# Attention, MoE, MoE: token rows scattered to one region per expert in place of a computed permutation

## The chip, the cores and the metric

The kernel is one program on one core of a Trainium2 chip. Its time is the time of one execution on the device, in microseconds (us). The engines are TensorE (PE; its weight loads are listed apart as PEld), VectorE (DVE), ScalarE (ACT), GpSimd (POOL) and SyncE (SP). They run their own instruction streams and meet at semaphores only. DMAs are issued from the streams of SP, ACT and POOL.

## The reference

All data are float32. N = 4 x 768 = 3072 tokens, DM = 8 heads x 64 = 512, E = 8 experts, F = 1024.

```python
x = attention(q, k, v)              # 4 batches, 8 heads; local window of 96, 8 global keys, a bias by distance
# first MoE
logits = x @ w_gate;  e = argmax(logits)
gate = softmax(logits)[e];  eom = sigmoid(x @ w_output_gate)[e]
x2 = gate * eom * (relu(x @ w1[e]) @ w2[e])
# second MoE
logits = normalise(x2) @ normalise(expert_emb).T / tau;  e = argmax(logits)
out = softmax(logits)[e] * (relu(x2 @ w1[e]) @ w2[e])
```

Each token goes to one expert, so the work of a layer is that of all token tiles (128 rows each), with every expert's count rounded up to whole tiles: 29 tiles in the first MoE and 28 in the second, for these inputs.

## The kernel before

**Attention.** The tokens are 24 tiles of 128 rows, six to a batch. `attention_steps` calls `step(b, u)` on PE, DVE and ACT, software-pipelined: 12 values of `u` for a batch, two for a tile (`j = u // 2`). The first batch's steps and the last ones are written out, batches 1 to 3 are a loop. In a step PE makes scores, transposes the probabilities, and multiplies them by V; DVE adds the bias (`nbias`) and takes the minimum; ACT takes the exponentials and copies transposed tiles. At the end of a tile PE transposes the sums (`x_transposes`) and multiplies by both gates (`gate_logits`), DVE normalises into `x_tok` (two buffers) and adds up the 16 logits of each token into `logits`, and ACT issues the store of the tile's rows to `x_rows` in DRAM (L727).

**Route.** After the last tile, `route` on DVE works on all tiles at once: the argmax as a one-hot array, counts, the gate weight of each token, each token's rank within its expert (PE, L1217 to L1221, with the triangular matrix `before` and with `ones`), and each token's place in the order by experts. That permutation is then inverted: 24 (second layer: 32) pairs of one-hot tiles go through PE (L1228), and what comes out is, for each slot, the token that it holds (`gather_i`), its scale (`scale_c`) and in the second layer the row that it is written to (`scatter_i`). `tab` holds the tile at which each expert ends.

**Experts.** The tiles then run expert by expert. For tile i: POOL gathers 128 rows by index into `x_g` (L632); PE transposes them (`x_tr`, L1126), DVE copies them to `x_gt` (L1064); `first_product` is 64 matmuls (L1246) into four banks, which ACT clears with ReLU into `h_t` (L777); `second_product` is 16 matmuls (L1256) into bank 4, which DVE scales into `y_sb` (L1075). The order on PE is

```python
first_product(i)       # waits for x_gt of tile i
x_tr(i + 1)
second_product(i)      # waits for h_t, and for y_sb of tile i - 1
```

so the transposition and the copy of the next tile lie under the second product. In the first layer ACT stores `y_sb` to `y_rows` and takes the squares for the norm, and DVE takes eight dot products with the expert embeddings (L1083, `next_logits`), from which `route` starts again. In the second layer POOL scatters `y_sb` to the output (L651). SP loads the weights: two experts are held at a time, and expert e + 2's first matrix is fetched as soon as expert e's last first product is done, its second one after the last second product.

Where a branch's condition fails (other sizes of the window), a general path with loops of its own is taken; it does not run here.

## Time and profile before

| | |
|---|---|
| median of 3 runs | 1151.79 us (1151.33 to 1152.15) |
| the profiled execution's own time | 1149.39 us |
| its span, first to last instruction | 1147.0 us |
| PE busy | 1061.3 us (93%) |
| DVE, ACT, POOL busy | 446.4, 262.9, 158.6 us |
| mean granted TensorE clock | 0.962 of full speed |

The profile is of one execution. The span is some 2 us shorter than the time that the device reports for it. A busy PE means that matmuls were in flight. Lines such as L1246 are lines of the kernel before.

### The profile page before, as it was taken

To read this page: it belongs to the slowest core of one execution; us is meant where nothing else is said; L and a number is where in the kernel's file an instruction comes from. 1 tells how busy PE (TensorE), PEld (TensorE's weight loads), DVE (VectorE), ACT (ScalarE), POOL (GpSimd) and SP (SyncE) were. 2 spreads that over 40 slices of the span, in tenths; PEclk is the share of its full clock that TensorE was granted. 3 is DMA by queue.
4 is the path that set the end of the run, shared out by engine and by line. 5 is a ranking of instruction groups with operands and counts; after the bars stand their busy time and mean duration, and the time that the engine had idled before them with its cause. 6 is when DMAs were issued, how large, how long until landed. Compare 5 with 4: busy or idle time off the path is not lost.

```text
span 1147.0 us, 20797 instructions
## 1 busy us (share of the span) xinstructions
PE 1061.3 (93%) x6936; PEld 806.0 (70%) x6936; DVE 446.4 (39%) x1541; ACT 262.9 (23%) x792; POOL 158.6 (14%) x437
## 2 busy tenths in 40 slices
PE   5999999848999999999999983799999999999995
PEld 4878888646777777777777763577777777777773
DVE  6777777662444444444444449100001111111110
ACT  4677677421111111111111110011111111111110
POOL 2010001001111111111111100122222222222221
PEclk9999999958999999999999995899999999999998
DMA  9865569211151542325151532015523235230110
GB/s 180 183 159 145 132 160 322 99 58 37 37 183 37 183 135 85 131 89 183 37 183 37 183 106 95 28 37 179 181 107 112 98 116 180 90 122 31 37 37 12
DMA packets 119861, 130.30 MB, mean 114 GB/s; under 512 B 80079, under 2 KB 80079, under 8 KB 119696
## 3 DMA queue, kind: packets, MB, share of 16 engines
q1 hardware_dynamic: 103456, 91.24, 26.8%
q0 software_dynamic: 6960, 21.77, 5.8%
q10 hardware_dynamic: 9408, 16.81, 4.0%
q8 instruction: 22, 0.36, 0.1%
q14 instruction: 15, 0.12, 0.0%
HBM read 103.58 MB, written 22.02 MB: 110 GB/s over the span
## 4 chain that ended last, share of the span: by engine, by line
PE 83%; issue 5%; DVE 5%; ACT 4%; DMA 1%; ACTq 1%; POOL 0%; POOLq 0%; DVEq 0%; SPq 0%
PE bank L1246 35%; PE bank L1256 34%; PE bank L1126 6%; PE bank L1199 2%; PE bank L1166 2%; PE bank L1228 2%; PE bank L1141 2%; ACT probs L709 2%; ACT q_t L687 1%; ACT y_two L721 1%; ACTq L727 1%; DVE neg_s L904 0%; DVE nbias L840 0%; DMA n_words<-in_n_local_dram 0%; DMA x_g<-x_rows,gidx 0%
## 5 line engine op out<-in xcount | busy, mean ns | idle before, releaser
L1246 PEld LDWEIGHTS bank<-x_gt,w_sb 128*128 128x128 f32 x3648 | 419.1, 193 | 28.7 <-issue 26.3
L1246 PE MATMUL bank<-x_gt,w_sb 128*128 128x128 f32 x3648 | 419.7, 276 | 1.6 <-DVE x_gt L1064 1.6
L1256 PE MATMUL bank<-w_sb,h_t 128*128 128x512 f32 x912 | 400.8, 592 | 0.0
L1256 PEld LDWEIGHTS bank<-w_sb,h_t 128*128 128x128 f32 x912 | 168.8, 190 | 190.8 <-issue 190.8
L777 ACT ACTIVATE h_t<-bank 128x256 f32<-128x256 f32 x228 | 86.8, 381 | 524.4 <-PE bank L1246 524.4
L1075 DVE TENSOR_SCALAR y_two<-bank,scale_c 128x512 f32<-128x512 f32 x57 | 42.8, 751 | 359.5 <-PE bank L1256 359.5
L586 POOL TENSOR_TENSOR pad_p<-zeros 128x1 f32<-128x1 f32 x196 | 36.9, 188 | 824.8 <-PE bank L1126 470.9
L1064 DVE COPY x_gt<-bank 128x512 f32<-128x512 f32 x59 | 40.8, 691 | 247.2 <-PE bank L1126 247.2
L1083 DVE CUSTOM_DVE_ANT_0 v_win<-y_two,nbias 128x512 f32<-128x512 f32 x174 | 108.8, 687 | 1.2
L785 ACT ACTIVATE y_two<-y_two 128x512 f32<-128x512 f32 x29 | 18.3, 631 | 246.4 <-DVE y_two L1075 246.4
L904 DVE CUSTOM_DVE_ANT_0 neg_s<-bank,nbias 128x256 f32<-128x256 f32 x192 | 70.3, 421 | 7.8 <-issue 6.0
L709 ACT ACTIVATE probs<-neg_s,neg_m 128x256 f32<-128x256 f32 x96 | 47.6, 497 | 51.1 <-DVE neg_m L904 51.1
L1166 PE MATMUL bank<-k_t,q_t 64*128 64x256 f32 x384 | 56.5, 414 | 2.7 <-DVE neg_m L904 1.5
L709 ACT ACTIVATE h_t<-neg_s,neg_m 128x256 f32<-128x256 f32 x96 | 47.7, 498 | 11.4 <-DVE neg_m L904 11.4
L1126 PE MATMUL bank<-ident,x_g 128*128 128x128 f32 x236 | 36.4, 278 | 14.9 <-DMA x_g<-y_rows,gidx 7.5
L1166 PEld LDWEIGHTS bank<-k_t,q_t 64*128 64x128 f32 x384 | 34.3, 192 | 13.7 <-issue 9.9
L1126 PEld LDWEIGHTS bank<-ident,x_g 128*128 128x128 f32 x236 | 28.2, 144 | 15.2 <-issue 15.2
L1083 DVE CUSTOM_DVE_ANT_0 q_in<-y_two,nbias 128x512 f32<-128x512 f32 x58 | 37.7, 687 | 0.0
L632 POOL DMA_INDIRECT x_g<-x_rows,gidx x30 | 31.4, 1045 | 16.0 <-issue 16.0
L632 POOL DMA_INDIRECT x_g<-y_rows,gidx x29 | 30.6, 1055 | 15.7 <-issue 15.7
L1126 PE MATMUL bank<-ident,probs 128*128 128x128 f32 x192 | 27.0, 285 | 5.9 <-ACT y_two L721 5.5
L1126 PEld LDWEIGHTS bank<-ident,probs 128*128 128x128 f32 x192 | 21.3, 144 | 15.6 <-ACT y_two L721 11.7
(176 smaller groups left out, 717.0 us busy)
## 6 DMA issues: line engine op xcount, KB each, us to landing
w_sb<-in_moe_w_dram SPq DMA_DIRECT2D x32, 2048.0 KB, 9.3
y_rows<-y_two ACTq DMA_DIRECT2D x29, 256.0 KB, 2.0
q_in<-in_q_dram SPq DMA_DIRECT2D x24, 256.0 KB, 3.8
k_in<-in_k_dram SPq DMA_DIRECT2D x24, 256.0 KB, 5.0
v_own<-in_v_dram SPq DMA_DIRECT2D x24, 256.0 KB, 3.4
x_rows<-x_tok ACTq DMA_DIRECT2D x24, 256.0 KB, 3.8
v_win<-v_own SPq DMA_DIRECT2D x20, 192.0 KB, 3.4
nbias<-in_moe_expert_emb_dram ACTq DMA_DIRECT2D x1, 2048.0 KB, 7.4
```

Of the source, the lines that this page charges most:

```text
L586: nc.gpsimd.tensor_tensor(pad_p[:, at:at + 1], zeros[:, 0:1], zeros[:, 0:1], ALU.add)
L632: nc.gpsimd.indirect_dma_start(out=x_g[:, :], out_offset=None, in_=src[:, :], in_offset=bass.IndirectOffsetOnAxis(ap=gidx[:, 0:1], axis=0) ...
L709: e_ = nc.scalar.activation(probs_of[u % 2][:, 2 * k + i, :], neg_s[:, k, i, :], ACT.Exp, bias=neg_m[:, i, s % STEPS:s % STEPS + 1], scale ...
L777: nc.scalar.activation(h_t[:, k * FPP:(k + 1) * FPP, :].rearrange("p c t -> p (c t)"), banks[k][:, 0:FPP * P], ACT.Relu).then_inc(L.h, 1)
L904: V.tensor_tensor_reduce(neg_s[:, k, i, :], score_banks[i][:, k * WIN:(k + 1) * WIN], nbias[:, c, 2 * (2 * half + k) + i, :], 1.0, 3e38, A ...
L1064: V.tensor_copy(x_gt[:, :, :].rearrange("p c t -> p (c t)"), banks[5][:, :]).then_inc(L.xt, 1)
L1075: V.tensor_scalar(y_sb, banks[4][:, :], scale_c[:, n, bass.ds(i, 1)], None, ALU.mult).then_inc(L.y, 1)
L1083: t_ = V.tensor_tensor_reduce(dot_out[e], y_sb, emb[:, e * DM:(e + 1) * DM], 1.0, 0.0, ALU.mult, ALU.add, dot[:, e:e + 1])
L1126: t_ = T.transpose(bank[:, c * P:(c + 1) * P], src[:, c * P:(c + 1) * P], ident[:, :])
L1166: m_ = T.matmul(score_banks[i][:, k * WIN:(k + 1) * WIN], q_t[rows, j % 2, 2 * half + k, :], k_t[rows, j % 2, 2 * half + k, :], start=True ...
L1246: m_ = T.matmul(banks[k][:, f * P:(f + 1) * P], w1_sb[:, w1 + c * FF + at:w1 + c * FF + at + P], x_gt[:, c, :], start=(c == 0), stop=(c == ...
L1256: m_ = T.matmul(banks[4][:, :], h_t[:, c, :], w2_sb[:, w2 + c * DM:w2 + (c + 1) * DM], start=(c == 0), stop=(c == FC - 1))
```

## The change

The rows of x are no longer stored in token order and gathered. DRAM has two arrays `bins` of one region (`CAP` rows) for each expert, and a row is 532 numbers: the 512 of x, then the token's scores and its number. While attention runs, DVE takes the argmax of three tiles at a time (`group_hot`), PE ranks their tokens (`group_ranks`), counting on from the groups before, and the rank plus the start of the expert's region is the row to which POOL scatters each token (`scatter_group`). The counts at the end give the tables (`tables`). Every region is filled up with zero rows behind its last token (`fill_bin`), and SP reads contiguous rows, in two DMAs of 64 rows for a tile. The scale of a tile's tokens is worked out when the tile is there, from the scores that came with its rows, on ACT (`gate_exps`) and DVE (`gate_weights`). In the first layer the same is done tile by tile for the next one: the scores are taken from the dot products (`next_scores`), PE ranks one tile (`rank_rows`), DVE makes the row numbers (`y_rows`) and POOL scatters (`bin_row`). The copy to `x_gt` moves from DVE to ACT, the loads of the weights from SP to ACT, and the expert loops of DVE and ACT are written out eight times, once for each expert. `route`, the permutation and the stores to `x_rows` and `y_rows` are gone.

The core of the diff (the general path, names and constants are left out):

```diff
+        def group_hot(dve, q, g, tile0):
...
+            link(V.tensor_scalar(own[:, :, ID_COL], ident_id[:, bass.ds(tile0, GROUP)], 0.0, None, ALU.add))
+            link(V.tensor_copy(g_pre[:, 0, :], g_pre[:, GROUP, :]))
+            link(V.tensor_reduce(g_min[:, :], neg, AX.X, ALU.min))
+            link(V.tensor_tensor(g_cmp[:, :, :], neg, wide(g_min[:, :]), ALU.is_equal))
+            link(V.tensor_tensor(g_cmp[:, :, :], g_cmp[:, :, :],
+                                 desc.unsqueeze(1).to_broadcast([P, GROUP, E]), ALU.mult))
+            link(V.tensor_reduce(g_min[:, :], g_cmp[:, :, :], AX.X, ALU.max))
+            link(V.tensor_tensor(g_hot[:, :, :], g_cmp[:, :, :], wide(g_min[:, :]), ALU.is_equal))
+            for m in range(GROUP):
+                ins = V.tensor_tensor(g_pre[:, m + 1, :], g_pre[:, m, :], g_hot[:, m, :], ALU.add)
...
+        def scatter_group(pool, hold_pool, q, g):
+            pool.wait_ge(s_pos, q + (1 + FIRST))
...
+            for m in range(GROUP):
+                nc.gpsimd.indirect_dma_start(
+                    out=bins[0][:, :], out_offset=bass.IndirectOffsetOnAxis(ap=sc_i[:, j:j + 1], axis=0),
+                    in_=x_tok[:, j, :], in_offset=None,
...
 # SP
+                for e in range(0, E, 2):
+                    fill_bin(sp, n, e)
+                def load_x(at, low, high):
+                    sp.wait_ge(L.xt, at + FIRST)
+                    sp.dma_start(x_g[0:UNIT, :], low).then_inc(L.x_ld, 16)
+                    sp.dma_start(x_g[UNIT:P, :], high).then_inc(L.x_ld, 16)
...
 # POOL, first layer
+                def bin_row(i):
+                    pool.wait_ge(L.y, i + (1 + FIRST))
+                    nc.gpsimd.tensor_copy(y_row[:, 0:DM], y_sb).then_inc(L.yc, 1)
+                    pool.wait_ge(L.yc, i + (1 + FIRST))
+                    pool.wait_ge(L.pos, i + (2 + FIRST))
...
 # ACT
-                t = j - 3
-                if half == 0 and exists(b, t, TPB):
-                    act.wait_ge(x_done, since(TPB * b + t + 1))
-                    act.dma_start(x_rows[bass.ds(b * S + t * P, P), :], x_tok[:, t % 2, :])\
-                        .then_inc(x_st[t % 2], 16)
...
+                def x_copy(i):
+                    act.wait_ge(L.x_ld, 32 * i + 32)
+                    act.wait_ge(L.t1, i + 1)
+                    act.wait_ge(L.mm1, MARKS * i + FIRST)
+                    act.wait_ge(L.sc, i + FIRST)
+                    nc.scalar.activation(pay[:, bass.ds(i + 1, 1), :].rearrange("p o c -> p (o c)"), x_g[:, DM:], ACT.Copy)
+                    nc.scalar.activation(x_gt[:, :, :].rearrange("p c t -> p (c t)"), banks[5][:, :],
+                                         ACT.Copy).then_inc(L.xt, 1)
...
+                for e, start, end in expert_spans(act, n):
+                    with act.Fori(start, end) as i:
+                        relu_full(i)
+                        gate_exps(i, e)
+                        x_copy(i + 1)
+                        if n == 0:
+                            squares(i)
+                    at = n * E + e + 2
+                    if at < 2 * E:
+                        act.wait_ge(L.mm1, MARKS * end + FIRST)
+                        load_w(act, at // E, at % E)
+                        act.wait_ge(L.mm2, end + FIRST)
+                        load_w2(act, at // E, at % E)
 # DVE (gate_weights, first layer)
+                        dve.wait_ge(L.ex, i + (1 + FIRST))
+                        chain(V.tensor_scalar(g_tmp4[:, 1:2], e_sum[:, :], 1e-9, None, ALU.add))
+                        chain(V.scalar_tensor_tensor(out=g_tmp4[:, 2:3], in0=e_sig[:, :], scalar=1.0,
+                                                     in1=g_tmp4[:, 1:2], op0=ALU.add, op1=ALU.mult))
+                    V.reciprocal(scale[:, :], g_tmp4[:, 2:3]).then_inc(L.sc, 1)
...
+                def y_rows(i):
+                    dve.wait_ge(L.rank, i + 1)
+                    ids = pay[:, bass.ds(i, 1), 2 * E:2 * E + 1].rearrange("p o c -> p (o c)")
+                    chain(V.tensor_tensor(cmp1[:, :], banks[6][:, 0:E], hot1[:, :], ALU.mult))
+                    chain(V.tensor_reduce(r1[:, 0:1], cmp1[:, :], AX.X, ALU.add))
+                    chain(V.tensor_scalar(r1[:, 1:2], ids, 0.0, OFF, ALU.is_equal, ALU.mult))
+                    V.tensor_tensor(sidx[:, :], r1[:, 0:1], r1[:, 1:2], ALU.add).then_inc(L.pos, 1)
...
+                for e, start, end in expert_spans(dve, n):
+                    with dve.Fori(start, end) as i:
+                        here(i)
+                        if n == 0:
+                            y_rows(i)
+                        gate_weights(i, e)
+                        y_full(i)
+                        if n == 0:
+                            next_scores(i)
...
 # PE
+                def rank_rows(i):
+                    pe.wait_ge(L.hot, i + FIRST)
+                    pe.wait_ge(L.pos, i + FIRST)
+                    T.matmul(banks[6][:, 0:E], before[:, :], hot1[:, :], start=True, stop=False)
+                    T.matmul(banks[6][:, 0:E], ones[:, :], pre1[:, :], start=False, stop=True).then_inc(L.rank, 1)
...
                     with pe.Fori(start, end) as i:
+                        first_full(i, w1)
                         x_tr(i + 1)
+                        second_full(i, w2)
+                        if n == 0:
+                            rank_rows(i)
```

`first_full` and `second_full` are the two products as they were. `L.sc` starts at `FIRST` (1) and rises by one for each tile's `gate_weights`; `L.rank` starts at 0. `chain` and `link` make DVE wait for its own instruction before the next one; in `chain` the value waited for is worked out from the loop's register.

## Rows read from the trace of the kernel before

**Rows 1.** The page: chain that ended last, shares by engine and line.

```profile
PE 83%; issue 5%; DVE 5%; ACT 4%; DMA 1%; ACTq 1%; POOL 0%; POOLq 0%; DVEq 0%; SPq 0%
```

**Rows 2.** Stretches: length, busy PE, PEld, DVE, ACT, POOL, clock, DMA share, GB/s.

```profile
150.00:180.00 30.00, 29.28 (x297) 24.40 (x292) 22.43 (x99) 20.30 (x69) 2.60 (x9) 1.00 0.63 151
...
226.00:244.00 18.00, 1.87 (x6) 1.78 (x6) 11.53 (x47) 7.86 (x20) 0.00 (x0) 0.51 0.33 133
...
280.00:685.00 405.00, 404.82 (x2353) 297.28 (x2351) 188.27 (x588) 59.99 (x168) 41.60 (x108) 1.00 0.33 114
```

**Rows 3.** Chain that ended last, whole kernel: start us, length us, what.

```profile
263.97 8.95 PE bank L1246 x64
...
540.32 7.14 PE bank L1246 x64
547.90 6.87 PE bank L1256 x16
...
677.95 6.88 PE bank L1256 x16
...
728.36 8.86 PE bank L1246 x64
```

**Rows 4.** The same chain, in the two gaps between the stages.

```profile
226.07 2.85 issue
...
231.72 2.47 issue
...
256.60 0.30 POOLq L625
...
258.38 3.62 DMA x_g<-x_rows,gidx
...
687.23 0.61 DVE v_win L1083
```

**Rows 5.** Timeline: small instructions and hand-overs, in and beside the gaps.

```profile
234.40 0.22 ACT L759 ACTIVATE r_rows<-r_rows 128x24 f32<-128x24 f32 x1 [4.11 <-DVE r_rows L965]
...
263.22 0.69 DVE L1064 COPY x_gt<-bank 128x512 f32<-128x512 f32 x1 [5.90 <-PE bank L1126]
...
701.38 0.43 PE L1221 MATMUL bank<-r_cum,ones 128*128 128x8 f32 x2
701.92 0.17 DVE L992 COPY r_t<-bank 128x8 f32<-128x8 f32 x1 [0.65 <-PE bank L1221]
...
703.10 0.17 DVE L999 TENSOR_TENSOR_SCAN r_tab<-r_t,zeros 128x8 f32<-128x8 f32 x1
703.31 0.17 DVE L1000 TENSOR_TENSOR r_t<-r_tab,r_t 128x8 f32<-128x8 f32 x1
```

**Rows 6.** Timeline: two steps of attention, inside the loop over batches.

```profile
153.61 0.34 ACTq L727 DMA_DIRECT2D x_rows<-x_tok  x1
...
155.44 0.06 DVE L902 MEMSET pad_v<- 128x1 f32 x1 [1.21 <-PE bank L1166]
...
158.07 0.28 DVE L883 TENSOR_TENSOR lg_part<-bank,inv_sum 128x128 f32<-128x128 f32 x1
...
158.49 0.37 DVE L887 TENSOR_REDUCE logits<-lg_part 128x128 f32 x1
...
160.13 0.06 DVE L902 MEMSET pad_v<- 128x1 f32 x1 [0.24 <-PE bank L1166]
```

**Rows 7.** Timeline: a gather issued by POOL beside an expert's tile.

```profile
404.69 1.04 POOL L632 DMA_INDIRECT x_g<-x_rows,gidx  x1 [0.53 <-issue]
```

**Rows 8.** ACT's copies of 128x512: duration ns, least, median, most.

```profile
L721 ACT ACTIVATE probs_t<-bank x24: 569/574/577, 21.9 to 217.6; 128x512 f32<-128x512 f32 x24
```

**Rows 9.** DMA issues: count, KB each, median us from issue to landing.

```profile
w_sb<-in_moe_w_dram SPq DMA_DIRECT2D x32, 2048.0 KB, 9.3
...
nbias<-in_moe_expert_emb_dram ACTq DMA_DIRECT2D x1, 2048.0 KB, 7.4
...
out_dram<-y_two,sidx POOLq DMA_INDIRECT x28, 2.7
```

More of the change, by code:

```diff
@@ L153, in attention_moe_moe @@
         dot = sb("dot", [P, E])
[L155 removed]
+        dot_out = [v_win[:, e, :] if e < TPB else k_in[:, e - TPB, :] for e in range(E)]
         tau_c = sb("tau_c", [P, 2])
@@ L612, in _ @@
+                for g in range(2):
+                    landed(pool, g, B)
             with pool.Else():
-                pool.wait_ge(s_flag, 1)
+                general_pool(pool, hold_pool)
+            pool.sem_inc(x_binned, 1)
             for n, L in enumerate(layers):
-                pool.wait_ge(L.perm, 1)
-                src, rows = (x_rows, N) if n == 0 else (y_rows, COLS * P)
-                if n == 0:
-                    pool.wait_ge(x_written, 1)
-                else:
-                    pool.wait_ge(layers[0].y_st, 16 * COLS + FIRST)
@@ L733, in _ @@
                 rows = slice(i * D, (i + 1) * D)
-                nc.scalar.activation(gates_h[rows, :, i, :], gates_w[rows, :, :], ACT.Copy).then_inc(s_gh, 1)
+                nc.scalar.activation(gates_h[rows, :, i, :], gates_w[rows, :, :], ACT.Copy,
+                                     scale=-1.0).then_inc(s_gh, 1)
+            act.wait_ge(s_const, 8)
+            for n in range(2):
+                act.dma_start(bins[n][ZERO:ZERO + UNIT, :], none[0:UNIT, :]).then_inc(zero_st, 16)
             act.wait_ge(s_flag, 1)
@@ L1104, in _ @@
+                if n == 0:
+                    here(end)
+                    y_rows(end)
             dve.wait_ge(s_flag, 1)
@@ L1213, in _ @@
             for n, L in enumerate(layers):
-                cols = NT if n == 0 else COLS
-                pe.wait_ge(L.counted, 1)
-                T.matmul(banks[0][:, 0:cols * E], before[:, :], r_oh[:, 0:cols, :].rearrange("p t e -> p (t e)"),
-                         start=True, stop=False)
-                T.matmul(banks[0][:, 0:cols * E], ones[:, :], r_cmp[:, 0:cols, :].rearrange("p t e -> p (t e)"),
-                         start=False, stop=True)
-                T.matmul(banks[1][:, 0:E], ones[:, :], r_cum[:, cols - 1, :], start=True, stop=True)\
-                    .then_inc(L.ranks, 1)
@@ L1223, in _ @@
-                nv = 2 + n
-                for t in range(cols):
-                    if t % CHUNK == 0:
-                        pe.wait_ge(L.onehot, t // CHUNK + 1)
-                    buf, at = slot_lo[t // LO_SPLIT], t % LO_SPLIT
-                    m_ = T.matmul(banks[2][:, 0:nv * COLS], buf[:, at * P:(at + 1) * P],
-                                  slot_hi[:, t, 0:nv, :].rearrange("p m g -> p (m g)"),
-                                  start=(t == 0), stop=(t == cols - 1))
-                m_.then_inc(L.perm_ps, 1)
+                if n == 0:
+                    pe.wait_ge(s_hot, NT // GROUP)
+                    pe.wait_ge(s_pos, NT // GROUP + FIRST)
+                    T.matmul(banks[7][:, 0:E], ones[:, :], g_pre[:, GROUP, :], start=True, stop=True)\
+                        .then_inc(L.counts, 1)
+                else:
+                    T.matmul(banks[7][:, 0:E], ones[:, :], pre1[:, :], start=True, stop=False)
+                    T.matmul(banks[7][:, 0:E], ones[:, :], hot1[:, :], start=False, stop=True).then_inc(L.counts, 1)
@@ L1260, in _ @@
                 x_tr(0)
-                start = 0
-                for e in range(E):
-                    end = pe.value_load(tab[0:1, n, e:e + 1], min_val=e + 1, max_val=TILES)
+                for e, start, end in expert_spans(pe, n):
+                    w1, w2 = e % 2 * KC * FF, e % 2 * FC * DM
                     pe.wait_ge(w1_ld[n][e % 2], 16 * (e // 2 + 1) + FIRST * (e % 2))
```

709 lines of the change are left out of this document (369 added, 340 removed).

## The prediction

> **What bounds the kernel now.** I read the chain of work that ended last first. Its shares say PE 83% [rows 1], so a change elsewhere counts only where PE waits for it. The stretches then show three kinds of time. In attention PE is busy 29.28 of 30 us at the full clock, with DVE and ACT at 22.4 and 20.3, so all three are close to the limit [rows 2]. In the first expert layer PE is busy 404.8 of 405 us [rows 2]: nothing else sets the pace there. Between them lies a stretch with PE busy 1.9 of 18 us at a clock of 0.51 [rows 2].
>
> The chain in order of time gives the sizes [rows 3]. A tile of an expert takes 7.14 us in the first product; 0.44 us later (the transposes) the second begins, of 6.87 us: 14.45 us with no hole. The first layer starts at 263.97 and ends at 677.95 + 6.88 = 684.83; the second starts at 728.36. Attention's last logits on DVE end at 226.0, just before the first piece of the gap [rows 4]. So there are two gaps: 38.0 us (226.0 to 263.97) and 43.5 us (684.83 to 728.36), 81.5 us in all. That is the most that removing the route could give. The diff puts part of that work inside attention and inside the tiles, so the question is whether it lies under PE there.
>
> **Inside the first layer's tiles: the term that decides.** I followed each wait from one tile to the next. On PE, `rank_rows(i)` stands behind the second product of tile i. On DVE, `y_rows(i)` waits for `L.rank` of i + 1, which starts at 0, so for just those matmuls; and it is the first thing in DVE's iteration, so `gate_weights(i)` stands behind it. On ACT, `x_copy(i + 1)` waits for `L.sc` of i + 1 + `FIRST`; with the credit of one that is i + 1 increments, the last of them from `gate_weights(i)`. PE's first product of tile i + 1 waits for that copy. In the kernel before, the copy lay under the second product. Now every tile ends in a loop PE, DVE, ACT, PE during which PE has nothing to do.
>
> Its price, from the moment at which the next first product would have started:
> - four small matmuls on PE. Two of 8 columns took 0.43 us at the lower clock [rows 5]; at the full clock I take 0.5 for the four;
> - 0.11 us from the matmul's end to DVE (701.81 to 701.92) [rows 5];
> - seven chained DVE instructions (four in `y_rows`, three in `gate_weights`) at 0.205 us from start to start (703.10 to 703.31) [rows 5]: 1.43;
> - two copies on ACT, 0.2 for the 20 columns (0.22 for 24 [rows 5]) and 0.57 for 128x512 [rows 8];
> - 0.06 to PE (263.91 to 263.97) [rows 3, 5].
>
> That is 2.87 us. In the loops the value that a wait needs is worked out in registers: between two DVE instructions in attention's loop 0.14 us pass (158.35 to 158.49) [rows 6] against 0.035 in straight code [rows 5]. Most of the seven are such, and some on ACT: 0.4 us more, 3.3 in all. The bounds are 2.9 (none of it seen) and 4.0 (0.15 on each). There are 28 steps from tile to tile: **+92 us** (81 to 112). The 29th lies in the second gap.
>
> The rest of the new work in a tile has cover. After the scale, DVE has the y copy and eight dot products at 0.61 us [rows 4], then seven small instructions, done some 10 us into a step of 17.7; PE asks for `hot1` at its end. POOL's scatter waits for the row numbers at the turn of the step and has the whole step.
>
> The loads of x_g need a word. SP may issue them when the copy to `x_gt` is done, and PE wants them after the first product, 7.1 us later. A gather of the same 256 KB landed after 3.62 us [rows 4]. Two halves, in parallel, take about 4.5 us with their issue and cost nothing, and I take that; two full-length ones in a row take 7.2 and some 0.8 of issue, which would put 0.9 us on each of 28 steps, up to +25. The Trainium skill, "DMA: Bandwidth & Descriptors", Rules for kernel authors, says of transfers to disjoint halves of the partitions that they serialize, since both use all 16 engines. By that page the halves gain nothing; taken as two half-length transfers they are still covered, taken as two full ones the sum would be the +25. No row here has two such loads.
>
> The weights are now issued by ACT after its last square, both matrices together. Of 2 MB each landed after 9.3 us [rows 9]; an expert has several tiles, so they are in time. ACT's ReLUs behind the issue have some 5 us of slack. For seven changes of expert I take +3 (0 to 14).
>
> **Attention.** For each three tiles DVE gets ten chained instructions in `group_hot`: 2.1 us at 0.21, or 3.1 with register waits. They stand before the scores of an odd step, for which DVE had idled 1.21 us [rows 6]: 0.9 to 1.9 late, I take 1.4. `group_rows` (three instructions, 0.6 to 0.9) stands before an even step with 0.24 idle [rows 6]: 0.4. PE gets four small matmuls: 0.4. That is 2.2 us, and PE, busy 29.28 of 30, can't catch up. Seven groups (the eighth is in the gap) make +15, with bounds 5 and 25. Against this ACT no longer issues the store, 0.34 us in its stream a tile [rows 6], which is on the path; PE's idle share (0.72 of 30) caps what that gives at 5 us over 208. POOL's scatter of three tiles, queued before `window` of the next tile, takes about 4.9 us (0.53 + 1.04 each [rows 7]) and starts early enough to leave 2 us. So **+10** (0 to 25). Five chained constants on DVE ahead of it: +1.
>
> **The first gap.** From the last logits: `group_hot` 2.1, ranks 0.9 at the lower clock, `group_rows` 0.6: 3.6. Then PE counts (0.9), one code load of 2.9 (the unexplained 2.85 and 2.47 [rows 4]), `tables` with nine instructions (1.8): 9.2. SP loads a register and issues a fill four times, at about 1.0 each (one register load is about 0.6 on POOL, 256.60 to the index copy at 257.20 [rows 4]): 13.2; one more register and two issues 1.4, landing 3.0, transposes 1.1, ACT's copies 0.85: 19.6. Two other branches end before it. POOL's three scatters are issued by 8.6 and land 2.7 us [rows 9] after the last issue began, at 10. On ACT the embeddings (7.4 [rows 9]) and eight squares end at 12, then four fills, 16. So 38.0 becomes 19.7: **-18** (-10 to -22).
>
> **The second gap.** Scale and row numbers 2.6, y 0.75, eight dots 4.9, seven small 1.75, with hand-overs 10.2; rank 1.0, `y_rows` 0.9, `tables` 1.8 and part of a code load 1.1: 15. SP's fills 4, register and issues 1.4, landing 3, transposes and copies 2: 25. 43.5 becomes 25: **-18.5** (-12 to -21). The last scatter (to 15.6) ends before the x load is issued.
>
> **The second layer.** There `gate_weights` waits for nothing at the end of the product. Its 18 instructions and ACT's exponential are done about 9 us into a tile, and `x_copy(i + 1)` with them, under the second product that covered it before: 0 (to +8). At the end one copy more: +0.5.
>
> **The sum.** 1 + 10 - 18 + 92 + 3 - 18.5 + 0.5 = +70. The profiled execution took 1149.4 us (span 1147.0) and becomes 1219; the median of the runs shown is 2.4 us above it: 1151.8 + 70 = **1222 us**.
>
> **The rivals.**
> - *The clock falls in every pause.* PE's longest pauses in attention are about 1 us and leave the clock at 1.00; in the gap, with pauses of 7 to 10 us, it was 0.51 [rows 2]. The new pause, near 3 us, lies between, and no row decides it. After a fall the first product took 8.95 instead of 7.14 [rows 3]: 1.8 x 28 = +50, 1272 us. The Trainium skill, "TensorE: Matmul & The Clock Gate", Why this matters for your kernels, advises against idle gaps between bursts of matmuls because they bring the clock back to half; by that page this rival is possible, and the trace agrees for the long gap (0.51).
> - *Code loads at each expert.* DVE's and ACT's loops are written out eight times. A load like the 2.85 and 2.47 [rows 4] on each of the 14 entries after the first, uncovered, gives 14 x 2.7 = +38, 1260 us. Against it: PE's loops are written out so already and show no hole, and the entries mostly have slack. The Trainium skill, "Runtime: NRT & Kernel Launch", Instruction fetch mechanics, says that a taken branch out of the fetched pages stalls; the trace agrees in so far as the two holes stand at new code.
> - *The pause isn't there, and the kernel gets faster.* If the wait of `x_copy` on the scale is met one tile earlier than I count (one credit more), the loop opens and the term of 92 shrinks to four matmuls, 28 x 0.43 = 12: 1142 us. It decides at a pause of 0.8 us a tile; below that the gaps win. For it speaks only that the waits are counted; by the code I find no second credit.
>
> **How the numbers follow.** My case 0.67 (own range 1200 to 1246), clock 0.16, code loads 0.08, no pause 0.04, the rest 0.05 (double-length x loads, for one). The other cases above reach 1260 and 1272; with the bounds of attention and the pause I put the top at 1277, and the bottom at 1195, where the low ends of pause, attention and gaps meet. Outside lie the no-pause case and stacked rivals. A measurement of this kernel tells no change from one of 0.2% (2.3 us). Faster by more: 0.05; within: 0.01; slower: 0.94.
>
> **What would show it.** In the first layer, a period of 17.4 to 18.4 us with PE waiting some 3 us for ACT's copy to `x_gt`, which follows DVE's scale; in the second layer still 14.45. Gaps of about 20 and 25 us. Attention some 10 us longer. Wrong it would be if the first layer's period were 14.9 (no pause) or if its first product took over 8 us (clock).

## The result, and the profile after

The changed kernel took 1236.28 us (median of 4 runs, 1229.99 to 1239.98) against 1151.97 (1151.33 to 1152.68) for the kernel before on the same chip: ratio 1.0726, 95% interval [1.0681, 1.0771], 84.3 us slower. Forecast were 1222 us, in a range of 1195 to 1277. The profiled execution took 1235.38 us with a span of 1233.5; before, the span was 1147.0, so 86.5 us are to be found in the trace.

The page of the changed kernel: its span, the chain that ended last, a group of instructions (busy, mean ns, idle before) and two DMA issues (KB each, us to landing).

```profile
span 1233.5 us, 23838 instructions
...
PE 44%; issue 34%; DMA 8%; DVE 4%; POOL 4%; ACT 3%; SPq 1%; POOLq 0%; another core or an unknown queue 0%; DVEq 0%; ACTq 0%
...
L1356 PE MATMUL bank<-x_gt,w_sb 128*128 128x128 f32 x3648 | 445.0, 286 | 67.5 <-ACT x_gt L886 67.5
...
w_sb<-in_moe_w_dram ACTq DMA_DIRECT2D x28, 2048.0 KB, 11.3
x_g<-bins SPq DMA_DIRECT2D x118, 133.0 KB, 2.9
```

PE had 83% of the chain before [rows 1] and now has 44%. The first product (L1246 before, L1356 now) stood idle 67.5 us for ACT's copy to `x_gt`; that wait is new.

Stretches of the changed kernel (length, busy PE, PEld, DVE, ACT, POOL, clock, DMA share, GB/s):

```profile
150.00:180.00 30.00, 28.45 (x287) 23.71 (x284) 22.07 (x100) 20.40 (x67) 8.25 (x18) 1.00 0.67 164
...
235.40:257.30 21.90, 2.68 (x10) 2.15 (x10) 5.33 (x30) 7.97 (x20) 3.13 (x4) 0.50 0.50 182
...
257.30:789.00 531.70, 461.41 (x2551) 346.97 (x2551) 239.77 (x952) 98.36 (x319) 72.86 (x110) 0.95 0.25 82
...
815.00:1221.00 406.00, 405.93 (x2352) 298.87 (x2352) 115.85 (x586) 67.90 (x225) 40.79 (x108) 1.00 0.29 96
```

Attention has PE busy 28.45 of 30 us where it was 29.28 [rows 2]. In the first expert layer PE, hardly ever idle before and at clock 1.00 [rows 2], is now idle 70 us and at a mean clock of 0.95. The second layer is as before.

By stage, with the borders of the prediction:

| stretch | before | after | change | predicted |
|---|---|---|---|---|
| to the last logits (attention, constants) | 226.0 | 235.4 | +9.4 | +11 |
| first gap | 38.0 | 21.9 | -16.1 | -18 |
| first layer | 420.9 | 531.7 | +110.8 | +95 |
| second gap | 43.5 | 26.1 | -17.4 | -18.5 |
| second layer and end | 418.6 | 418.4 | -0.2 | +0.5 |

**One turn from tile to tile**, timeline of the changed kernel (start, length, engine, line, what, idle before and its releaser):

```profile
383.14 0.37 PE L1342 MATMUL bank<-pre,ones 128*128 128x8 f32 x2
383.55 0.17 DVE L1165 TENSOR_TENSOR cmp<-bank,hot 128x8 f32<-128x8 f32 x1 [8.02 <-PE bank L1342]
...
384.25 0.16 DVE L1168 TENSOR_TENSOR sidx<-r 128x1 int32<-128x1 f32 x1
384.35 0.15 DVE L1137 TENSOR_SCALAR g_tmp<-e_sum 128x1 f32<-128x1 f32 x1
...
384.74 0.16 DVE L1140 RECIPROCAL scale<-g_tmp 128x1 f32<-128x1 f32 x1
...
385.08 0.22 ACT L885 ACTIVATE pay<-x_g 128x20 f32 x1 [8.44 <-DVE scale L1140]
385.21 0.58 ACT L886 ACTIVATE x_gt<-bank 128x512 f32<-128x512 f32 x1
...
385.84 0.60 PE L1356 MATMUL bank<-x_gt,w_sb 128*128 128x128 f32 x3 [2.33 <-ACT x_gt L886]
```

Ranks on PE to 383.51, seven instructions on DVE to 384.90, two copies on ACT to 385.79, PE again at 385.84: the loop of the prediction, link by link. DVE had idled 8.02 us and ACT 8.44 before it; neither lacks time, only the order makes them late. From the end of the second product to the next first product 2.68 us pass, 2.33 of them with PE idle. The turn costs 2.94 us, the plain period being 17.39 against 14.45: without a pause the first product starts 0.16 us before the second one ends and takes 7.31 us, behind a pause it takes 7.41.

But 28 x 2.94 = 82 and the layer lost 110.8. The granted clock has most of the rest. Here are two pauses and the beginnings of the two first products behind them, as stretches:

```profile
290.90:294.20 3.30, 1.04 (x6) 0.60 (x4) 1.85 (x10) 0.69 (x3) 0.73 (x2) 1.00 0.00 0
294.30:297.30 3.00, 3.00 (x27) 3.00 (x28) 3.00 (x11) 1.45 (x3) 0.37 (x1) 1.00 0.63 182
308.30:311.60 3.30, 1.03 (x6) 0.60 (x4) 1.86 (x10) 0.69 (x3) 0.74 (x2) 1.00 0.00 0
311.70:314.70 3.00, 3.00 (x20) 3.00 (x21) 3.00 (x11) 0.95 (x3) 0.37 (x1) 0.73 0.61 182
```

The pauses are alike (PE busy 1.04 and 1.03 of 3.30 us). Behind the first the clock stays at full speed; behind the second it falls to the lower of its two levels for a time (mean 0.73), PE gets 20 matmuls done instead of 27, and the first product takes 9.04 instead of 7.41 us. In this execution 13 of the 28 turns fell; nine of these products took 9.04 us, three 8.75 to 8.80, and one 10.36. Above 7.41 they add up to 21.7 us, and the first tile, 9.56 instead of 8.95, adds 0.6. (The group L1356 was busy 238.8 us in this layer against 213.6 before, 25.2 more; 2.8 of that are 28 times the 0.1 that is in the 2.94 already.)

The last part stands at the changes of expert. Timeline of the second one:

```profile
403.33 0.40 ACTq L598 DMA_DIRECT2D w_sb<-in_moe_w_dram  x1
403.37 0.47 SPq L671 DMA_DIRECT2D x_g<-bins  x1
...
403.83 0.45 ACTq L603 DMA_DIRECT2D w_sb<-in_moe_w_dram  x1
404.03 0.48 SPq L672 DMA_DIRECT2D x_g<-bins  x1
...
411.74 0.44 PE L1231 MATMUL bank<-ident,x_g 128*128 128x128 f32 x2 [1.09 <-DMA x_g<-bins]
```

ACT issues 4 MB of weights in the same microsecond in which SP issues the two halves of the next x rows; PE's transposes wait 1.09 us for the rows. Such waits come to 4.5 us, and to 6.1 with what each draws after it (the second product then starts some 0.2 us later still, and the three turns behind the second change have pauses of 2.40 to 2.65). The parts, 82.3 + 21.7 + 0.6 + 6.1 = 110.7, meet the 110.8. Waits of note stand at four of the seven changes; at the other three the first product beside the loads was one of the long ones, which hid them.

The first gap, in the chain that ended last ("issue" is a hole that waits for nothing in the profile; SPq L541 is a table read, L671 a load of x rows):

```profile
240.01 2.21 issue
...
244.29 0.57 SPq L541
...
251.87 0.58 SPq L671
...
252.67 2.63 DMA x_g<-bins
```

### The profile page after: what moved, and what is told of

It reads as the page before. It is cut to its first block, busy times and chain, and to the rows that moved or that the text cites. A ratio compares the mean times of both kernels' runs of the same rounds, so it can differ in the third digit from the quotient of the medians.

```text
span 1233.5 us, 23838 instructions
## 1 busy us (share of the span) xinstructions
PE 1083.6 (88%) x6970; PEld 825.5 (67%) x6970; DVE 553.8 (45%) x2432; ACT 324.1 (26%) x1052; POOL 168.7 (14%) x353
## 4 chain that ended last, share of the span: by engine, by line
PE 44%; issue 34%; DMA 8%; DVE 4%; POOL 4%; ACT 3%; SPq 1%; POOLq 0%; another core or an unknown queue 0%; DVEq 0%; ACTq 0%
PE bank L1356 17%; PE bank L1366 16%; DMA bins<-q_in,sidx 8%; PE bank L1231 5%; POOL q_in L768 2%; PE bank L1273 2%; PE bank L1311 2%; POOL pad_p L718 2%; PE bank L1247 1%; ACT probs L831 1%; DVE neg_s L1041 1%; ACT y_two L843 1%; ACT q_t L809 1%; ACT k_t L817 1%; DMA n_words<-in_n_local_dram 0%
## 5 line engine op out<-in xcount | busy, mean ns | idle before, releaser
L1356 PE MATMUL bank<-x_gt,w_sb 128*128 128x128 f32 x3648 | 445.0, 286 | 67.5 <-ACT x_gt L886 67.5
L1356 PEld LDWEIGHTS bank<-x_gt,w_sb 128*128 128x128 f32 x3648 | 439.2, 202 | 83.7 <-ACT x_gt L886 70.8
L1165 DVE TENSOR_TENSOR cmp<-bank,hot 128x8 f32<-128x8 f32 x30 | 5.0, 167 | 279.7 <-PE bank L1342 279.7
L885 ACT ACTIVATE pay<-x_g 128x20 f32 (+1 forms) x59 | 12.9, 219 | 300.4 <-DVE scale L1140 266.6
L1154 DVE CAST sidx<-r 128x1 int32<-128x1 f32 x28 | 4.3, 154 | 166.3 <-PE bank L1366 166.3
L831 ACT ACTIVATE h_t<-neg_s,neg_m 128x256 f32<-128x256 f32 x96 | 47.6, 497 | 22.9 <-DVE neg_m L1041 22.9
L1134 DVE TENSOR_SCALAR g_tmp<-e_sum 128x1 f32<-128x1 f32 x28 | 4.3, 154 | 96.7 <-ACT d_out L906 96.7
L1175 DVE CUSTOM_DVE_ANT_0 k_in<-y_two,nbias 128x512 f32<-128x512 f32 x58 | 44.9, 812 | 0.0
L1159 DVE TENSOR_SCALAR y_two<-bank,scale 128x512 f32<-128x512 f32 x57 | 42.8, 751 | 2.0
L886 ACT ACTIVATE x_gt<-bank 128x512 f32<-128x512 f32 x59 | 34.1, 578 | 0.0
```

The lines of the kernel that those rows point to most:

```text
L831: e_ = nc.scalar.activation(probs_of[u % 2][:, 2 * k + i, :], neg_s[:, k, i, :], ACT.Exp, bias=neg_m[:, i, s % STEPS:s % STEPS + 1], scale ...
L886: nc.scalar.activation(x_gt[:, :, :].rearrange("p c t -> p (c t)"), banks[5][:, :], ACT.Copy).then_inc(L.xt, 1)
L1159: V.tensor_scalar(y_sb, banks[4][:, :], scale[:, :], None, ALU.mult).then_inc(L.y, 1)
L1175: t_ = V.tensor_tensor_reduce(dot_out[e], y_sb, emb[:, e * DM:(e + 1) * DM], 1.0, 0.0, ALU.mult, ALU.add, dot[:, e:e + 1])
L1356: m_ = T.matmul(banks[k][:, f * P:(f + 1) * P], w1_sb[:, w1 + c * FF + at:w1 + c * FF + at + P], x_gt[:, c, :], start=(c == 0), stop=(c == ...
```

## The experiments

Each ratio is against the kernel before, run on the same chip in turn with it.

**The pause: its cause.** Two kernels leave the work of the changed kernel as it is and take the scale off the way to the next tile. In the first, DVE works the scale out ahead of the row numbers:

```diff
                     with dve.Fori(start, end) as i:
                         here(i)
+                        gate_weights(i, e)
                         if n == 0:
                             y_rows(i)
-                        gate_weights(i, e)
                         y_full(i)
```

> On the changed kernel, DVE works out a tile's scale before it waits for the tile's ranks; nothing else is changed. Theory A (the loop ranks, row numbers, scale, copy, first product opens the pause; the clock falls in some of the pauses): the copy to x_gt goes back under the second product, a first-layer tile takes 14.45 + 0.43 (the four small matmuls) = 14.9 us, its first product 7.1 us in every tile but the first, and the time is 1236.3 - 110.8 + 12 = about 1138 us, below the kernel before. Theory B (the tiles are slower for another reason: the small matmuls drain PE, or the loads of x or of the weights come late): a tile stays above 17 us and the time above 1215 us.

Measured: 1144.08 us (1142.70 to 1144.33), ratio 0.994 [0.9923, 0.9956]. The period is 14.90 us in most steps, the first product 7.39. Behind changes of expert it is up to 15.86, and the first tile's is 17.41, where the kernel below has 16.60. Its second gap is 29.0 us, where the kernel below has 25.9, and that is the largest part of the 4.9 us between the two. Why this order loses there I did not follow further; the forecast that the two agree within 3 us failed.

In the second, ACT's wait for the scale stands where its reason is, at `gate_exps`, and no longer in `x_copy`:

```diff
 # x_copy
                     act.wait_ge(L.mm1, MARKS * i + FIRST)
-                    act.wait_ge(L.sc, i + FIRST)
...
 # gate_exps, first layer
                         act.wait_ge(L.xt, i + (1 + FIRST))
+                        act.wait_ge(L.sc, i + FIRST)
```

> On the changed kernel, ACT's wait for the scale of the tile before moves from the copy to x_gt to the exponentials of the next tile; DVE's order stays as it is. Theory A: the same loop is opened at another link, so tiles of about 14.9 us and about 1138 us, as in the run with DVE's order changed, within 3 us. If DVE's order is itself the cost (the y copy and the scores late behind the ranks, whatever the copy does): the time stays above 1160 us.

Measured: 1139.21 us (1136.90 to 1140.01), ratio 0.9899 [0.9882, 0.9916]. ACT's copy, and PE 6 us later, in two stretches of its timeline:

```profile
281.05 0.58 ACT L885 ACTIVATE x_gt<-bank 128x512 f32<-128x512 f32 x1
...
287.50 0.37 PE L1342 MATMUL bank<-pre,ones 128*128 128x8 f32 x2
...
287.73 0.47 PE L1356 MATMUL bank<-x_gt,w_sb 128*128 128x128 f32 x2
```

The copy lies under the second product again; only the ranks are left in the turn. All 27 periods behind the first tile are 14.90 (272.83 to 675.04). One line moved takes 97 us off the changed kernel, more than the pause itself: the fallen clock and the late x rows went with it. The sum closes from the other side too. To the last logits it is +9.1, the gaps are -16.8 and -17.6, the first layer is +12.6 (28 x 0.45 for the ranks), the second with the end +0.6: -12.1, and the span shrank by 12.1.

**The pause put into the kernel before.** All else as before, but DVE scales y before it copies the next `x_gt`:

```diff
-                x_copy(1)
+                if n == 1:
+                    x_copy(1)
...
+                    x_copy(1)
...
-                    x_copy(i + 1)
+                    if n == 1:
+                        x_copy(i + 1)
...
+                        x_copy(i + 1)
```

> On the kernel before, DVE scales y before it copies the next tile to x_gt, in the first layer; nothing else is changed. One link of the changed kernel's loop, alone: 0.3 to DVE, 0.75 for y, 0.7 for the copy, 0.06 to PE, about 1.7 to 1.8 us of pause behind each of 28 tiles, with no small matmuls. Theory A with a clock that falls only in longer pauses: a period of 16.2 us, +49 us, 1201 us. If the clock falls in pauses of 1.8 us as well, as it does behind half of those of the changed kernel: 1225 to 1245 us. If a pause of this size is absorbed: 1152 us.

Measured: 1208.70 us (1208.01 to 1209.98), ratio 1.0504 [1.0487, 1.0522], 57.5 us slower. One of its turns:

```profile
315.73 7.41 PE L1250 MATMUL bank<-x_gt,w_sb 128*128 128x128 f32 x64 [1.75 <-DVE x_gt L1064]
```

The period is 16.45 to 16.48 us from the second turn on, 28 x 2.0 = +56. The pause itself was forecast rightly (1.7 to 1.8); the turn costs 0.26 more, as above. So a copy behind the second product costs this much without any of the new layout. And here the first product takes 7.41 in all 28 turns: behind 27 pauses of 1.73 to 1.76 us, and one of 1.44, the clock never fell.

**The clock.** Two wide matmuls on `ident`, into a bank that is free, behind the ranks. They fill all but 0.7 us of the pause, compute nothing that is used, and leave the loop of waits as it is:

```diff
                         if n == 0:
                             rank_rows(i)
+                            for _ in range(2):
+                                T.matmul(banks[7][:, 0:456], ident[:, :], iota_f[:, 0:456], start=True, stop=True)
```

> On the changed kernel, two matmuls of 128x456 into an unused bank follow the ranks in every first-layer tile: about 1.6 us of PE work in a pause of 2.33 us, behind everything that the loop waits for. They add nothing to the result. If the long first products (8.9 instead of 7.1 us, in 16 of 28 tiles) are the granted clock that falls in the pause: the clock stays at 1.00, every first product but the first takes 7.1 us, the period is 17.4 us throughout, and the time falls by 26 to 28 us to about 1209 us. If they are long for another reason (memory traffic, loads of weights), or if PE needs the pause: 1236 us or more.

Measured: 1215.76 us (1215.53 to 1219.19), ratio 1.0570 [1.0552, 1.0589]. Every first product behind the first tile took 7.41 us, at clock 1.00, and the plain period is 17.39 as in the changed kernel. One of them:

```profile
310.60 7.41 PE L1356 MATMUL bank<-x_gt,w_sb 128*128 128x128 f32 x64 [0.70 <-ACT x_gt L886]
```

PE's useless work saves 20.5 us, and the runs lie 3.7 us apart instead of 10.0. That is below the 26 to 28 I had expected: the fallen clock was worth 21.7, and with all first products short the x rows come late at all seven changes of expert, 8.4 us in place of 6.1. The pause of the loop is thus worth what it costs at full clock, and the fallen clock comes on top.

The other direction, a longer loop, with seven more chained instructions of one column in `gate_weights`:

```diff
+                        for _ in range(7):
+                            chain(V.tensor_scalar(g_tmp4[:, 3:4], g_tmp4[:, 2:3], 1.0, None, ALU.mult))
                     V.reciprocal(scale[:, :], g_tmp4[:, 2:3]).then_inc(L.sc, 1)
```

> The changed kernel with seven more chained DVE instructions of one column in `gate_weights` of the first layer, between the sum of exponentials and the reciprocal, so inside the loop PE, DVE, ACT, PE. My theory (PE stands still for the whole of that loop): the pause for `x_gt` grows from 2.3 us by seven times 0.2 to 3.7 us, 28 times, +39 us. For the clock two cases: if it is the length of the pause that lets it fall, it now falls in all 28 steps, not in some 14, another +22 us (1295); if something else picks the steps, the same ones are slow, 1275. Rival (the instructions of DVE have cover): period still 17.4, time 1236.

Measured: 1297.03 us (1295.51 to 1297.48), ratio 1.1270 [1.1253, 1.1286]. A first product, and the stretches of the pause ahead of it and of its first 3 us:

```profile
318.57 9.04 PE L1358 MATMUL bank<-x_gt,w_sb 128*128 128x128 f32 x64 [3.65 <-ACT x_gt L886]
```

```profile
314.90:318.50 3.60, 0.02 (x1) 0.00 (x0) 2.93 (x17) 0.69 (x3) 1.20 (x2) 1.00 0.08 33
318.60:321.60 3.00, 3.00 (x18) 3.00 (x19) 3.00 (x9) 0.57 (x2) 1.49 (x2) 0.64 0.43 126
```

The pause is 3.65 us, 1.32 longer, which makes 37 us: DVE's instructions stand on the path one for one. And now all 28 first products take 9.04 us or more (9.04 to 9.79), 15 turns beyond the 13, at 1.63 us each: 24 us. Together 61; measured 60.8, where luck helps, for the longer falls here (+2.4) and the x rows, which are hardly late any more (-5.7), are in neither. Pauses of up to 1.76 us never let the clock fall, those of 2.33 (2.68 with the ranks) let it fall in some turns and not in others, those of 3.65 (4.00) in all. Which turns fall at 2.33 is not settled: two that look alike differ. Nor does length alone decide between kernels: at the start of attention PE idled 2.44 us in the changed kernel, and the clock fell (0.50 from 19.5 to 22.9 us), and 2.69 us at the same place with the moved wait, and it did not. The Trainium skill, "TensorE: Matmul & The Clock Gate", Why this matters for your kernels, advises against idle gaps between bursts of matmuls; the traces agree for the pauses of 2.33 and 3.65 us, and those of 1.75 cost no clock. A number of falls that differs from run to run would also explain the spread of the changed kernel: between its fastest run (mean clock 0.962) and its slowest (0.953) lie 10 us, which would be six turns. Only one of these runs has a trace, so that is an estimate.

**The late x rows.** On top of the kernel with the wide matmuls, ACT holds the weights back until the next x rows have landed:

```diff
                     if at < 2 * E:
                         act.wait_ge(L.mm1, MARKS * end + FIRST)
-                        load_w(act, at // E, at % E)
                         act.wait_ge(L.mm2, end + FIRST)
+                        if e < E - 1:
+                            act.wait_ge(L.x_ld, 32 * end + 64)
+                        load_w(act, at // E, at % E)
                         load_w2(act, at // E, at % E)
```

> The kernel with the two wide matmuls behind the ranks (clock held, 1215.8 us), and ACT's issue of the two weight matrices held back until the next rows of x have landed (one more wait on their semaphore). My theory (the 4 MB of weights, issued in the same microsecond as the x rows, share the DMA engines with them and make them late): the idle of 0.4 to 1.5 us before the transposes at the seven changes of expert goes, and the period there falls to 17.4: -5 to -6.5 us. Rival (the x rows are late by their own table read on SP, the first load of an expert): no change. A second cost could show: ACT held 3 us at the change, its ReLUs late.

Measured: 1208.46 us (1207.89 to 1211.38), ratio 1.0506 [1.0492, 1.0519], 7.3 us below the kernel with the wide matmuls. The waits of 0.4 to 1.5 us at the seven changes are gone: behind the first turn the period is 17.39 or 17.40 in 24 of 27, and 17.45 to 17.71 in the three behind the second change. The reading of the weights as the cause holds.

And with one DMA of 128 rows for two of 64, the weights not held:

```diff
-                    sp.dma_start(x_g[0:UNIT, :], low).then_inc(L.x_ld, 16)
-                    sp.dma_start(x_g[UNIT:P, :], high).then_inc(L.x_ld, 16)
+                    sp.dma_start(x_g[:, :], both).then_inc(L.x_ld, 16)
... (the loop's source rows and the values waited for follow)
```

> The same kernel with the two wide matmuls, with the rows of x read by one DMA of 128 rows instead of two of 64. If halves on disjoint partitions run one behind the other at the same total, nothing changes in the plain steps (both are covered, 17.4 us), one issue less on SP (some 0.6 us) and landing near 3 us; at the changes of expert the transposes wait as long as before or up to 0.6 us less each (0 to -4 us). If a DMA of 128 rows took half as long as two of 64, the waits at the changes would fall by 1 us or more each (-6).

Measured: 1209.38 us (1207.29 to 1209.81), ratio 1.0504 [1.049, 1.0517], 6.4 below: at the high end of what I had called possible, and I had not seen why. DMA issues (KB each, median us to landing) at the second change of expert, first with two halves, then with one load:

```profile
w_sb<-in_moe_w_dram ACTq DMA_DIRECT2D x2, 2048.0 KB, 16.1
x_g<-bins SPq DMA_DIRECT2D x2, 133.0 KB, 6.7
```

```profile
w_sb<-in_moe_w_dram ACTq DMA_DIRECT2D x2, 2048.0 KB, 15.3
x_g<-bins SPq DMA_DIRECT2D x1, 266.0 KB, 4.9
```

The weights are issued at the same moment in both. SP needs some 0.67 us from one issue to the next, and in the meantime ACT has issued the second matrix; the second half then comes in behind 4 MB. It decides: the first half lands 6.1 us after its issue (at 404.5 us), before PE asks for the rows (405.6), the second 7.4 us after its own (406.4), and PE waits 0.79. The single load is issued before the second matrix, lands in 4.9 us, and PE wants it after 7.2. The order of issue is not all of it: the first half is issued at the same distance from both matrices as the single load, is half as large, and yet took 1.2 us longer. No run here shows why. The Trainium skill, "DMA: Bandwidth & Descriptors", Rules for kernel authors, advises one transfer over 128 partitions in place of two to disjoint halves; this run agrees, with 6.4 us at seven changes of expert, and nothing in the other 21 steps, where either way is covered. Its section Issuing engines are not separate DMA queues says that transfers started by different engines share the same 16 DMA engines and interleave; the 6.7 us beside the weights against 2.9 elsewhere agree.

**Attention.** Into the kernel before, at every third tile, ten chained DVE instructions of 24 columns where the changed kernel has `group_hot`; in the second run three more, a step later, where it has `group_rows`. Nothing else of the change:

```diff
+                t = u - 10
+                if t % 6 == 0 and exists(b, t // 6, 2):
+                    q = 2 * b + t // 6
+                    for n_ in range(10):
+                        V.tensor_scalar(r_tmp[:, 0:24], col[:, 0:24], 1.0, None, ALU.mult).then_inc(g_link, 1)
+                        dve.wait_ge(g_link, 13 * q + (n_ + 1))
+                t = u - 11
+                if t % 6 == 0 and exists(b, t // 6, 2):
+                    q = 2 * b + t // 6
+                    for n_ in range(10, 13):
+                        V.tensor_scalar(r_tmp[:, 0:24], col[:, 0:24], 1.0, None, ALU.mult).then_inc(g_link, 1)
+                        dve.wait_ge(g_link, 13 * q + (n_ + 1))
```

> The kernel before, whole route and all, with ten more chained DVE instructions of 24 columns at every third tile of attention, where the changed kernel has `group_hot`, and nothing else of the change. My theory (DVE has 1.2 us to spare there at most): 2 us of work, 0.8 to 1.4 us of it on the path, some seven times: +6 to +10 us, and attention ends that much later. Rival (DVE's work lies under PE): within 1 us of before; then the +9.4 us of attention come from PE's small matmuls or from POOL's scatters.

> The kernel before with the ten chained DVE instructions at every third tile of attention and three more in the step behind them, where the changed kernel has `group_rows`. Of the 9.4 us that attention took more in the changed kernel, 1.8 stand ahead of the first scores and ten instructions made 4.0; 3.7 are left. My theory (the three of `group_rows` stand before a step without slack, 0.24 us idle): 0.4 to 0.6 us for each of seven groups, +3 to +4 on top of the ten, about 1158.5. Rival (they are covered too, and the rest comes from DVE waiting in `group_rows` for the ranks of PE, or from POOL's scatters): below +1 on top, 1155 to 1156.

Measured: with ten 1155.11 us (1153.98 to 1158.84), ratio 1.0043 [1.0029, 1.0056]; with thirteen 1161.55 (1160.25 to 1163.31), ratio 1.0088 [1.0072, 1.0104]. The last logits on DVE, with ten and with thirteen:

```profile
229.61 0.37 DVE L887 TENSOR_REDUCE logits<-lg_part 128x16 f32<-128x128 f32 x1
```

```profile
235.00 0.37 DVE L887 TENSOR_REDUCE logits<-lg_part 128x16 f32<-128x128 f32 x1
```

They ended at 226.0 before. Ten instructions, 2 us of work at each of seven groups, moved the end by 4.0 us; three more moved it by another 5.4. The ten stand before a step for which DVE idles 1.21 us, the three before one with 0.24 [rows 6]. So what instructions cost here depends on where they stand, not only on how many there are. But 5.4 us are 0.8 a group, more than the 0.6 that the three take themselves, and they were only measured on top of the ten, one step behind them; no run has the three alone.

> The same kernel with the moved wait, with the two small f32 matmuls of `group_ranks` in attention issued twice for each three tiles. Attention takes 9.4 us more than before, ten chained DVE instructions alone explained 4.0 of it. My theory (PE is at its limit, so its matmuls count in full): 0.4 to 0.5 us for each of seven groups, attention +3 us, total +3. Rival (they fall into PE's small holes there, which are 0.7 of 30 us): below +1, and the missing 5 us come from `group_rows`, the scatters or the constants.

The edit, on the kernel with the moved wait:

```diff
 # group_ranks: the two matmuls, and once more
+            T.matmul(banks[5][:, rank_cols], ones[:, :], g_pre[:, 0:GROUP, :].rearrange("p t e -> p (t e)"),
+                     start=False, stop=True)
+            T.matmul(banks[5][:, rank_cols], before[:, :], g_hot[:, :, :].rearrange("p t e -> p (t e)"),
+                     start=True, stop=False)
```

Measured: 1137.94 us (1137.38 to 1138.55), ratio 0.9886 [0.9870, 0.9901], against 0.9899 [0.9882, 0.9916] without. PE is busy 196.7 instead of 194.1 us from 20 to 222 us, and attention does not end later. My theory fell: PE, busy 97% of that stretch before and 96% with the moved wait, was not what set the pace here; its small holes took the matmuls.

**What is left in the tile, and a version that beats both.** On the kernel with the moved wait, the operands of `rank_rows` in bf16, in which these whole numbers are exact:

```diff
-        hot1 = sb("hot1", [P, E])
-        pre1 = sb("pre1", [P, E])
+        hot1 = sb("hot1", [P, E], mybir.dt.bfloat16)
+        pre1 = sb("pre1", [P, E], mybir.dt.bfloat16)
...
-                    T.matmul(banks[6][:, 0:E], before[:, :], hot1[:, :], start=True, stop=False)
-                    T.matmul(banks[6][:, 0:E], ones[:, :], pre1[:, :], start=False, stop=True).then_inc(L.rank, 1)
+                    T.matmul(banks[6][:, 0:E], before_h[:, :], hot1[:, :], start=True, stop=False)
+                    T.matmul(banks[6][:, 0:E], ones_h[:, :], pre1[:, :], start=False, stop=True).then_inc(L.rank, 1)
```

> The kernel with the moved wait (1139.2 us), where a tile still takes 14.90 us against 14.45 before, with the operands of `rank_rows` (`hot1`, `pre1` and copies of `before` and `ones`) in bf16, in which these whole numbers below 256 are exact. My theory (the 0.45 us a tile are the four passes of the two small f32 matmuls on PE, the only thing left on the path): a quarter of the passes, period about 14.6, 28 x 0.3 = -8 us, 1131. Rival (the 0.45 is hand-over at the turn of the step, whatever stands there): period still 14.9, no change.

Measured: 1127.04 us (1125.86 to 1128.03), ratio 0.9789 [0.9776, 0.9803]. Its turn:

```profile
287.23 0.17 PE L1346 MATMUL bank<-hot,before_h 128*128 128x8 bf16 x1
287.26 0.17 PE L1347 MATMUL bank<-pre,ones_h 128*128 128x8 bf16 x1
287.28 0.91 PE L1361 MATMUL bank<-x_gt,w_sb 128*128 128x128 f32 x6
```

The period falls to 14.59 (272.69 to 287.28): 28 x 0.31 = -8.7 us, and from the start of one layer to that of the other the traces differ by 8.4 (459.4 and 451.0). The medians differ by 12, the spans of the profiled executions by 9.2: the one was the fastest of its four runs (1136.90), the other the slowest of its five (1128.03). The expectation of 8 us goes by the traces. Last, with one DMA for the x rows as well:

> The moved wait, the ranks in bf16, and the rows of x read by one DMA of 128 rows instead of two of 64. If my reading holds, the loads are covered in both expert layers, and one issue less on SP shortens only the two gaps, by some 0.7 us each: 1 to 2 us below the kernel with the ranks in bf16 alone, about 1129 to 1130. If loads are part of the period somewhere, more.

Measured: 1126.56 us (1125.74 to 1128.27), ratio 0.9788 [0.9775, 0.9801]: not to be told from the one before it. In the expert layers either way of loading is covered when nothing else is late. The 1 to 2 us that I expected from the gaps are not there: the gaps are 21.1 and 25.5 us, against 20.9 and 25.6 with two halves. Both versions are 2.1% faster than the kernel before (2.0 to 2.2% by the intervals), with the new layout whole.

## Why the prediction was right, and where it was off

- **The loop at the turn of a tile** was the right mechanism, and the waits that close it were read rightly: moving one opened it, lengthening it by seven instructions lengthened the pause by 1.32 us. The price of a turn was 2.94 us, not 3.3, and 82 us instead of 92. The 0.4 for waits on register values hardly exists. That 2.87, the sum without it, comes so near is partly luck: the links that it adds up took 2.68, and the other 0.26, the overlap of the two products that a pause takes away, was not in it.
- **The clock** was the mis-sized term. I set two cases, never and in every pause, and gave the second 0.16. The truth lay between: 13 of 28 turns, 21.7 us. With a pause between those taken to be harmless (about 1 us; in attention the trace has up to 0.67 in the running part and 1.5 at the start, at clock 1.00) and those known to fell the clock (7 us), a share of the turns should have stood in the sum; half of the +50 would have been near, though no row could have told the share. The 1.8 us for a fall compared products of two kinds, 8.95 behind a gap and 7.14 in the chain; behind a pause it was 9.04 against 7.41, so 1.63.
- **Changes of expert**: forecast +3 for ReLUs behind the issue of weights; measured 6.1 us in the changed kernel, and 7.3 where holding the weights took it away with the clock held, from another cause. I had compared the landing of the x rows with the tile (covered, and it is) and that of the weights with the expert (in time, and they are), but never set the two beside each other on the same engines in the same microsecond.
- **Attention**: +10 forecast, and with +1 for constants 11 in all; measured 9.4. The total was right, the terms were not. Ten instructions cost 0.6 us a group, not 1.4; three more, where `group_rows` stands, 0.8, not 0.4; four more small matmuls on PE nothing, not 0.4. The first scores came 1.8 us later than before, not 1. That makes 4.0 + 5.4 + 1.8 = 11.2, so some 2 us came back; the store that ACT no longer issues is the likely place, but it was only argued. POOL's scatters in attention were not tested by themselves.
- **The gaps**: 21.9 us for 19.7 and 26.1 for 25. One hole of 2.2 us ahead of `tables`, where a code load of 2.9 was forecast, was there; that it is a code load is argued from its place at new code. SP's part was too short: from the table (244.29) to the first load of x rows (251.87) 7.6 us, where 4.6 were counted.
- **The second layer**: nothing, as forecast. **Code loads at each expert**: false, no entry shows one on the path; with the moved wait all 27 periods, changes of expert included, are 14.90. **No pause**: false; but that rival gave 1142 us for the open loop, and the kernels that open it took 1139 and 1144.
- **Luck**: 1236.3 lies inside the range that I gave to my case alone, the one in which the clock does not fall, and yet it fell in 13 turns. The pause taken 10 us too dear hid part of the 22 us of clock. In the first layer the errors are -9.7 for the pause, +22.3 for the clock with the first tile, and +3.1 for the changes of expert.

## What to carry to other kernels

When work on the critical engine is handed through two others and back, look for the wait that closes the loop: it need not be long work, only work behind the wrong instruction, and the cure can be one line (here, one wait moved: 97 us). Price a new pause of the matmul engine twice, once as time and once as what the clock does behind it. And when a load moves to another queue, put its issue beside those of all other queues in the same microsecond; two halves of a transfer give the others a place to come between (6.4 us here).

## What the runs showed that I had not expected

- The granted clock fell behind none of 28 pauses of 1.44 to 1.76 us, 13 of 28 of 2.33 us (three of them 2.40 to 2.65), and all 28 of 3.65 us. Most falls made the first product 1.63 us longer (7.41 to 9.04), one 2.95. Two stretches with the same 1.03 or 1.04 us of work in 3.30 us could differ.
- Two wide matmuls whose result nobody reads, in such a pause, saved 20.5 us and most of the spread between runs.
- PE busy 29.28 of 30 us [rows 2] did not mean that four small matmuls more cost anything in attention, while three DVE instructions of 0.2 us, on top of ten a step earlier, cost 0.8 us at the step before which DVE had had 0.24 us to spare.
- 133 KB landed after 2.9 us away from the weights and after some 7 when issued behind 4 MB of them from another queue. Beside the same weights a load of 266 KB landed after 4.9 us, and the first of two halves, issued at the same distance from them, after 6.1.
